# Attention on one core: the row reciprocals' path (transpose, copy, store, broadcast load) is reordered

## The chip, the cores and the metric

The kernel runs on 1 core of one Trainium2 chip. The metric is the device time of one execution in microseconds (us). The core has TensorE (PE; its weight loads are listed as PEld), VectorE (DVE), ScalarE (ACT), GpSimd (POOL) and SyncE (SP), which here only issues DMAs. PSUM is the memory that TensorE writes to, in banks of 512 fp32 columns; SBUF is the working memory. Engines run their own instruction lists in order and wait for each other by semaphores.

## What is computed

```python
def _attn_ref(q, k, v):                      # B, H, S, D = 4, 8, 576, 64
    scores = scale * q @ k^T
    mask = (pos[:, None] // 64) >= (pos[None, :] // 64)     # causal in blocks of 64
    scores = where(mask, scores, -1e9); scores -= max(scores, -1)
    attn = exp(scores)
    attn = attn / (sum(attn, -1) + 1e-9)
    return attn @ v
...
x = attn_out.transpose(0, 2, 1, 3).reshape(2304, 512)
x = elu(x @ w_in) @ w_out                    # d_ff = 2048
x = x + top-1 mixture of 8 experts (d_ff = 1024), for the tokens whose skip score is positive
```

The change lies in attention alone. The two feed-forward stages follow after it and aren't touched.

## The kernel before, in words

Attention handles the 32 heads as 16 pairs; the two heads of a pair lie one above the other in the 128 partitions. The 576 rows of a head are four row tiles of 128 (u = 0 to 3) and a tail of 64; the two tails of a pair together are the fifth tile (u = 4, `LAST`). The scores of tile u go to PSUM (`s_ps`), VectorE takes their negated maxima (`row_max`, L332, L335), ScalarE writes the exponentials to `prob` with their row sums in `rowsum` (`exp`, L456), TensorE transposes `prob` into `t_ps` (`turn_pair`, `turn_head`, `turn_last`, `turn_corner`, all recorded at L533), VectorE copies the result to `pt` (L342, L350, L356, L363), and TensorE multiplies `pt` with v into `o_ps` (`values`, L584). `o_ps` has the head's columns in its partitions and the 576 rows in its columns, not yet divided by the row sums.

The division needs each row's reciprocal along the columns, the same in 64 partitions. It is made so: ScalarE adds 1e-9 to the nine columns of sums (`guard`, L463), VectorE takes the reciprocals (`recips`, L373, tile `recip`, 128 x 9), TensorE transposes them together with the corner of the last tile into columns 384 to 511 of bank 0 of `t_ps` (`turn_pair` of the next pair, u = 0), VectorE copies them to `r_rows` (9 x 128, L368), SyncE stores these rows to `recip_rows` in device memory (`store_recips`, L218) and loads them back, broadcast over 64 partitions each, with four DMAs to `r_sb` (`load_recips`, L224, L227). VectorE then multiplies `o_ps` with `r_sb` into `attn_sb` (`final`, L379), and SyncE stores that (`store`, L211).

Work is software-pipelined over pairs. All engines have a `step(kk, i)` for pair `now` = n, in which they also do late parts of `past` = n-1 and `older` = n-2 and the preparation of `after` = n+1. Steps for pairs 0, 1, 14 and 15 and two closing steps are unrolled, the others are in a loop with two steps per turn. Each engine's list in a step is fixed by hand:

- TensorE: scores 0 and 1 of now; head tiles u = 3 of past; second half of values of older; the transposes of q's, of the tails', and (after the scores of u = 2) of k's tiles of after (`prep`, L492, groups 0, 1, 2, into banks 0, 1, 0 of `t_ps`); `turn_last` of past (bank 1); scores 3; `turn_pair` u = 0 (bank 0, with past's corner and reciprocals) and u = 1 (bank 1); scores of the last tile; first half of values of past; head tiles u = 2.
- VectorE: maxima 0 and 1; copies of past's head tiles u = 3; `recips(past)`; `final(older)`; maxima 2; `turned_last`; maxima 3; `turned_corner` and the copy to `r_rows`; `turned_pair` 0 and 1; maxima of the last tile; copies of head tiles u = 2.
- ScalarE: exponentials 0 and 1; copies of q's, the tails' and k's transposes to `qk_f` (`prep_copy`, L437, L442 and L444, L439); exponentials 2, 3 and last; `guard`.
- SyncE: load v (3 DMAs); store `attn_sb` of older; store the rows of past; load q and k of pair n+3 (6 DMAs); load `r_sb` of past (4 DMAs); load a piece of w_in.
- GpSimd splits q and k of after into high and low parts, then w_in's piece.

Where a text gives times inside a step, the reader can find each group by its line, operation and tile.

## Time and profile before

| | us |
|---|---|
| median of 3 runs | 856.7 (855.65 to 857.85) |
| the profiled execution | 859.39 |
| its span, first to last instruction | 857.7 |
| PE busy in the span | 804.7 (94%) |
| DVE busy | 531.8 (62%) |
| ACT busy | 340.1 (40%) |
| POOL busy | 241.4 (28%) |
| mean granted TensorE clock, share of full | 0.983 |

Attention takes the first 224 us of the span. The kernel behind it is on TensorE. Busy shares of the whole span are means over stages with different limits, so attention has to be read by itself, in its own windows: which engine waits there, for whom, and what stands behind the waiting instruction in its list. Idle time of an engine that isn't the bound costs nothing. Ends of matmuls are modelled, and their starts are the safer number. "Idle before <- releaser" is inferred from semaphore events.

### The profile page before, as it was taken

To read this page: it belongs to the slowest core of one execution; us is meant where nothing else is said; L and a number is where in the kernel's file an instruction comes from. 1 tells how busy PE (TensorE), PEld (TensorE's weight loads), DVE (VectorE), ACT (ScalarE), POOL (GpSimd) and SP (SyncE) were. 2 spreads that over 40 slices of the span, in tenths; PEclk is the share of its full clock that TensorE was granted. 3 is DMA by queue.
4 is the path that set the end of the run, shared out by engine and by line. 5 is a ranking of instruction groups with operands and counts; after the bars stand their busy time and mean duration, and the time that the engine had idled before them with its cause. 6 is when DMAs were issued, how large, how long until landed. Compare 5 with 4: busy or idle time off the path is not lost.

```text
span 857.7 us, 14746 instructions
## 1 busy us (share of the span) xinstructions
PE 804.7 (94%) x4618; PEld 665.6 (78%) x4619; DVE 531.8 (62%) x1318; ACT 340.1 (40%) x815; POOL 241.4 (28%) x232
## 2 busy tenths in 40 slices
PE   5998899999599999999999999999997999999995
PEld 4665666666598998898898888888985777887884
DVE  3766667677333358758848848843765799376342
ACT  3655546554133232232232222222443387255141
POOL 2756556554254202102102102100011233122121
PEclk9999999999699999999999999999999899999998
DMA  6344544553422421120021020050241599355100
GB/s 144 101 120 134 143 126 132 147 156 96 153 63 72 145 84 31 47 83 20 10 75 28 9 75 1 26 195 3 79 160 57 169 308 352 143 179 178 31 26 8
DMA packets 102913, 88.10 MB, mean 103 GB/s; under 512 B 66676, under 2 KB 78340, under 8 KB 102736
## 3 DMA queue, kind: packets, MB, share of 16 engines
q1 hardware_dynamic: 99808, 82.48, 31.1%
q0 software_dynamic: 3056, 5.00, 1.8%
q8 instruction: 26, 0.43, 0.2%
q14 instruction: 23, 0.19, 0.1%
HBM read 72.26 MB, written 18.34 MB: 106 GB/s over the span
## 4 chain that ended last, share of the span: by engine, by line
PE 69%; DVE 2%; issue 1%; DVEq 1%; ACT 0%; POOL 0%; POOLq 0%; ACTq 0%
PE h_ps L1563 11%; PE out_ps L1563 11%; PE h_ps L1564 11%; PE h_ps L1565 11%; PE out_ps L1565 11%; PE out_ps L1564 11%; PE out_ps L1698 1%; PE tr_ps L1663 1%; PE lg_ps L1614 1%; DVEq L864 0%; DVE xt_lo L1271 0%; PE tr_ps L1603 0%; DVE ht_lo L1310 0%; DVE x2t L1300 0%; DVE tile_ids L1280 0%
## 5 line engine op out<-in xcount | busy, mean ns | idle before, releaser
L1401 ACT ACTIVATE ex<-h_ps 128x384 f32<-128x384 f32 x96 | 47.2, 492 | 278.1 <-PE h_ps L1565 278.1
L1563 PE MATMUL h_ps<-xt_hi,wi_hi 128*128 128x384 f32 x384 | 133.4, 347 | 8.2 <-DVE xt_lo L1271 8.2
L1564 PE MATMUL h_ps<-xt_lo,wi_hi 128*128 128x384 f32 x384 | 131.4, 342 | 0.0
L1565 PE MATMUL h_ps<-xt_hi,wi_lo 128*128 128x384 f32 x384 | 131.2, 342 | 0.0
L1239 DVE TENSOR_SCALAR ex<-ex 128x384 f32<-128x384 f32 x96 | 34.8, 363 | 146.7 <-ACT ex L1401 145.6
L1563 PE MATMUL out_ps<-wo_hi,gt 128*128 128x512 f32 x288 | 114.6, 398 | 0.0
L1565 PE MATMUL out_ps<-wo_hi,gt 128*128 128x512 f32 x288 | 113.9, 395 | 0.0
L1564 PE MATMUL out_ps<-wo_lo,gt 128*128 128x512 f32 x288 | 113.3, 393 | 0.0
L456 ACT ACTIVATE prob<-s_ps,negmax 128x128 f32<-128x128 f32 (+2 forms) x144 | 77.9, 548 | 83.9 <-DVE negmax L332 74.3
L1121 DVE CUSTOM_DVE_ANT_0 x2t<-x,w_raw 128x512 bf16<-128x512 f32 x108 | 82.8, 807 | 0.4
L1563 PEld LDWEIGHTS h_ps<-xt_hi,wi_hi 128*128 128x128 f32 x384 | 73.3, 191 | 12.2 <-DVE xt_lo L1271 8.8
L1564 PEld LDWEIGHTS h_ps<-xt_lo,wi_hi 128*128 128x128 f32 x384 | 73.5, 191 | 3.1
L533 PE MATMUL t_ps<-ident,prob 128*128 128x128 f32 (+1 forms) x400 | 61.0, 284 | 15.1 <-DVE pt L356 14.4
L1565 PEld LDWEIGHTS h_ps<-xt_hi,wi_lo 128*128 128x128 f32 x384 | 73.4, 191 | 0.0
L1027 POOL DMA_INDIRECT route_table<-entry,slot x18 | 20.9, 1164 | 177.2 <-DVE slot L1200 161.0
L1019 POOL TENSOR_TENSOR xt_lo<-x_raw,xt_hi 128x384 fp32r<-128x384 f32 x20 | 28.4, 1419 | 142.7 <-ACT xt_hi L1415 142.6
L533 PEld LDWEIGHTS t_ps<-ident,prob 128*128 128x128 f32 (+1 forms) x400 | 42.2, 140 | 29.7 <-DVE pt L356 17.6
L1565 PEld LDWEIGHTS out_ps<-wo_hi,gt 128*128 128x128 f32 x288 | 54.1, 188 | 13.4
L1563 PEld LDWEIGHTS out_ps<-wo_hi,gt 128*128 128x128 f32 x288 | 54.1, 188 | 9.2 <-DVE gt L1232 0.8
L1564 PEld LDWEIGHTS out_ps<-wo_lo,gt 128*128 128x128 f32 x288 | 54.1, 188 | 8.9
L332 DVE TENSOR_REDUCE negmax<-s_ps 128x2 f32<-128x256 f32 (+1 forms) x64 | 51.1, 819 | 11.7 <-PE s_ps L528 11.5
L293 POOL TENSOR_TENSOR qk_hi<-qk_f,one 128x512 fp32r<-128x512 f32 (+1 forms) x30 | 36.0, 1199 | 79.1 <-PE s_ps L528 58.7
(174 smaller groups left out, 1647.1 us busy)
## 6 DMA issues: line engine op xcount, KB each, us to landing
w_raw<-in_moe_w_dram SPq DMA_DIRECT2D x56, 512.0 KB, 5.6
attn_t<-attn_sb SPq DMA_DIRECT2D x16, 288.0 KB, 2.1
x_raw<-attn_t SPq DMA_DIRECT2D x24, 192.0 KB, 2.7
out_dram<-x SPq DMA_DIRECT2D x18, 256.0 KB, 2.2
x_rows<-x SPq DMA_DIRECT2D x18, 256.0 KB, 2.5
raw_qk<-in_q_dram SPq DMA_DIRECT2D x32, 128.0 KB, 2.4
raw_qk<-in_k_dram SPq DMA_DIRECT2D x32, 128.0 KB, 2.4
v<-in_v_dram SPq DMA_DIRECT2D x32, 128.0 KB, 2.7
```

The lines of the kernel that those rows point to most:

```text
L293: pool.tensor_tensor(qk_hi[i][:, a:b], qk_f[i][:, a:b], one[:, :].to_broadcast([P, b - a]), ALU.mult).then_inc(split_hi, 1)
L332: dve.tensor_reduce(heads_cols(negmax, u), s_pair(u), AX_X, ALU.max, negate=True).then_inc(max_done, 1)
L456: act.activation(dst, src, ACT.Exp, bias=negmax[:, c:c + 1], accum_out=rowsum[i][:, c:c + 1]).then_inc(exp_done, 1)
L533: return pe.transpose(t_ps[0:src.shape[1], bank, at:at + P], src, ident[:, :])
L1019: pool.tensor_tensor(xtk(b % 2, 1, k), x_raw[k][:, :], xtk(b % 2, 0, k).bitcast(F32), ALU.subtract).then_inc(x_lo_done, 1)
L1027: pool.indirect_dma_start(table, bass.IndirectOffsetOnAxis(ap=slot[j][:, 0:1], axis=0), entry[j][:, :], None, bounds_check=E * N - 1, oob_ ...
L1121: ins = dve.tensor_tensor_reduce(dot_rows[:, ((E + 1) * t + e) % 2], x2[s][:, :], all_skip if e == E else all_gates[:, e, :], 1.0, 0.0, AL ...
L1239: dve.tensor_scalar(e, e, 1.0, -1.0, ALU.min, ALU.add).then_inc(em_done, 1)
L1401: act.activation(ex[:, f % 2], h_ps[:, f % 2, 0:NB], ACT.Exp).then_inc(ex_done, 1)
L1563: pe.matmul(dst, stat[0], mov[0], start=start, stop=False, skip_group_check=True)
L1564: pe.matmul(dst, stat[0], mov[1], start=False, stop=False, skip_group_check=True)
L1565: return pe.matmul(dst, stat[1], mov[0], start=False, stop=stop, skip_group_check=True)
```

## The change

The rows of reciprocals get a place of their own. TensorE transposes `recip` right behind the tails' transposes (`turn_recips`, into columns 128 to 255 of bank 1 of `t_ps`), for which it first waits for `rec_done`. ScalarE copies them to `r_rows` (`recip_rows`) between the copies of the tails' and of k's transposes; VectorE's copy is gone. The tails' `prep_copy` waits for the transposed reciprocals (`r_turned`) in place of the tails' own transposes, and `turn_last`, which overwrites bank 1, waits for ScalarE's copy (`r_row_done`). On SyncE the rows of past are stored ahead of `attn_sb` of older and loaded ahead of q and k. The rows in device memory are two buffers that alternate.

```diff
--- before.py
+++ after.py
@@ -75,9 +75,10 @@
     O0 = BANK - O_SPLIT
     COLS = 2 * FULL + 1
     TURNS = 7
+    R_LOADS = 64
     PIECES = [(j, max(j * P, a), b) for j in range(T) for a, b in ((0, O_SPLIT), (O_SPLIT, S)) if j * P < b]
     PARTS = [PIECES[0:4], PIECES[4:]]
-    R0 = BANK - P
+    R0 = P
 
     with ExitStack() as ctx:
         def sb(name, shape, dt):
@@ -108,7 +109,7 @@
         half_row = sb("half_row", [P, P], BF16)
         mask_row = sb("mask_row", [P, CAUSAL], BF16)
 
-        r_dram = nc.dram_tensor("recip_rows", (COLS, P), F32, kind="Internal").ap()
+        r_dram = [nc.dram_tensor(f"recip_rows{i}", (COLS, P), F32, kind="Internal").ap() for i in range(2)]
 
         s_ps = ctx.enter_context(nc.psum_tensor("s_ps", [P, 4 * BANK], F32))
         t_ps = ctx.enter_context(nc.psum_tensor("t_ps", [P, 2, BANK], F32))
@@ -128,6 +129,7 @@
         turned = sem("turned")
         guard_done = sem("guard_done")
         rec_done = sem("rec_done")
+        r_turned = sem("r_turned")
         r_row_done = sem("r_row_done")
         r_stored = sem("r_stored")
         r_in = sem("r_in")
@@ -211,20 +213,20 @@
                 sp.dma_start(attn_t[bass.ds((n % GROUP) * P, P), bass.ds((n // GROUP) * S, S)],
                              attn_sb[i][:, :]).then_inc(stored[i], 16)
 
-            def store_recips(n):
-
+            def store_recips(n, i):
 
                 wait(sp, r_row_done, n + 1)
-                sp.dma_start(r_dram, r_rows[:, :]).then_inc(r_stored, 16)
-
-            def load_recips(n):
+                sp.dma_start(r_dram[i], r_rows[:, :]).then_inc(r_stored, 16)
+
+            def load_recips(n, i):
+
                 wait(sp, r_stored, 16 * n + 16)
                 for h in range(2):
                     rows = slice(h * D, (h + 1) * D)
-                    sp.dma_start(r_sb[rows, 0:FULL * P], r_dram[h * FULL:(h + 1) * FULL, :]
+                    sp.dma_start(r_sb[rows, 0:FULL * P], r_dram[i][h * FULL:(h + 1) * FULL, :]
                                  .rearrange("(o u) q -> o (u q)", o=1).broadcast_to([D, FULL * P]))\
                       .then_inc(r_in, 16)
-                    sp.dma_start(r_sb[rows, FULL * P:S], r_dram[COLS - 1:COLS, rows]
+                    sp.dma_start(r_sb[rows, FULL * P:S], r_dram[i][COLS - 1:COLS, rows]
                                  .broadcast_to([D, TAIL])).then_inc(r_in, 16)
 
             def load_wi(n):
@@ -236,14 +238,14 @@
                 n, _ = pair(kk, i)
                 if not (isinstance(n, int) and n < 2):
                     load_v(n, i)
+                if (past := pair(kk, i, -1)):
+                    store_recips(*past)
                 if (older := pair(kk, i, -2)):
                     store(*older)
-                if (past := pair(kk, i, -1)):
-                    store_recips(past[0])
+                if past:
+                    load_recips(*past)
                 if (ahead := pair(kk, i, 3)):
                     load_qk(*ahead)
-                if past:
-                    load_recips(past[0])
                 if (after := pair(kk, i, 1)):
                     load_wi(after[0])
 
@@ -265,9 +267,9 @@
             for kk in (NK - 2, NK - 1):
                 for i in range(2):
                     step(kk, i)
+            store_recips(PAIRS - 1, 1)
             store(PAIRS - 2, 0)
-            store_recips(PAIRS - 1)
-            load_recips(PAIRS - 1)
+            load_recips(PAIRS - 1, 1)
             store(PAIRS - 1, 1)
             for i in range(2):
                 sp.wait_ge(stored[i], 16 * NK)
@@ -364,8 +366,6 @@
                                       t_ps[0:TAIL, 0, 2 * P:3 * P].rearrange("p (h w) -> p h w", h=2))
                 if last:
                     ins.then_inc(turned, 1)
-                wait(dve, r_stored, 16 * n)
-                dve.tensor_copy(r_rows[:, :], t_ps[0:COLS, 0, R0:R0 + P]).then_inc(r_row_done, 1)
 
             def recips(n):
 
@@ -374,7 +374,7 @@
 
             def final(n, i):
                 wait(dve, pv_done, n + 1)
-                wait(dve, r_in, 64 * n + 64)
+                wait(dve, r_in, R_LOADS * (n + 1))
                 wait(dve, stored[i], 16 * (n // 2))
                 dve.tensor_tensor(attn_sb[i][:, :], o_ps[:, O0:O0 + S], r_sb[:, :], ALU.mult)\
                    .then_inc(out_done, 1)
@@ -427,7 +427,11 @@
         def _(act):
             def prep_copy(n, i, g, bank):
 
-                wait(act, prep_t, 3 * n + g + 1)
+
+                if g == 1 and not (isinstance(n, int) and n < 2):
+                    wait(act, r_turned, n - 1)
+                else:
+                    wait(act, prep_t, 3 * n + g + 1)
                 if g == 0:
                     wait(act, split_lo, 2 * (n - 1))
                 if isinstance(n, int) and n == 0 and g == 0:
@@ -462,6 +466,12 @@
                 wait(act, rec_done, n)
                 act.activation(guarded[:, :], rowsum[i][:, :], ACT.Copy, bias=1e-9).then_inc(guard_done, 1)
 
+            def recip_rows(n):
+
+                wait(act, r_turned, n + 1)
+                wait(act, r_stored, 16 * n)
+                act.activation(r_rows[:, :], t_ps[0:COLS, 1, R0:R0 + P], ACT.Copy).then_inc(r_row_done, 1)
+
             for g in range(3):
                 prep_copy(0, 0, g, (0, 1, 0)[g])
 
@@ -473,6 +483,10 @@
                     if after:
                         prep_copy(*after, 0, 0)
                         prep_copy(*after, 1, 1)
+                if past:
+                    recip_rows(past[0])
+                if now:
+                    if after:
                         prep_copy(*after, 2, 0)
                     exp(*now, 2)
                     exp(*now, 3)
@@ -543,13 +557,11 @@
                         wait(pe, prep_out, 3 * ahead[0] + 3)
                     else:
                         wait(pe, turned, turns(n - 1, 3, 0))
-                    wait(pe, rec_done, n)
                 for h in range(2):
                     for j in range(c):
                         last = turn(u, (h * c + j) * P, prob[u][h][:, j * P:(j + 1) * P])
                 if u == 0 and past:
-                    turn(0, 2 * P, prob4[:, FULL * P:S])
-                    last = turn(0, R0, recip[:, :])
+                    last = turn(0, 2 * P, prob4[:, FULL * P:S])
                 last.then_inc(pt_done, 1)
 
             def turn_head(n, u, h):
@@ -560,9 +572,9 @@
                     last = turn(h, j * P, prob[u][h][:, j * P:(j + 1) * P])
                 last.then_inc(pt_done, 1)
 
-            def turn_last(n, ahead):
+            def turn_last(n):
                 wait(pe, exp_done, exps(n, LAST, 0))
-                wait(pe, *((prep_out, 3 * ahead[0] + 2) if ahead else (turned, turns(n, 3, 1))))
+                wait(pe, r_row_done, n + 1)
                 for j in range(FULL):
                     last = turn(1, j * P, prob4[:, j * P:(j + 1) * P])
                 last.then_inc(pt_done, 1)
@@ -570,9 +582,10 @@
             def turn_corner(n):
 
                 wait(pe, turned, turns(n, 3, 0))
-                wait(pe, rec_done, n + 1)
-                turn(0, 2 * P, prob4[:, FULL * P:S])
-                turn(0, R0, recip[:, :]).then_inc(pt_done, 1)
+                turn(0, 2 * P, prob4[:, FULL * P:S]).then_inc(pt_done, 1)
+
+            def turn_recips(n):
+                turn(1, R0, recip[:, :]).then_inc(r_turned, 1)
 
             def values(n, i, part):
                 wait(pe, turned, turns(n + 1, 0) if part else turns(n, LAST))
@@ -607,15 +620,20 @@
                 if after:
                     wait(pe, turned, turns(past[0], 3, 0)) if past else pe.wait_ge(prep_out, 3)
                     prep(*after, 0, 0)
-                    wait(pe, turned, turns(past[0], 3, 1)) if past else pe.wait_ge(prep_out, 3)
+                if past:
+                    wait(pe, turned, turns(past[0], 3, 1))
+                    wait(pe, rec_done, past[0] + 1)
+                if after:
                     prep(*after, 1, 1)
+                if past:
+                    turn_recips(past[0])
                 if now:
                     scores(*now, 2)
                 if after:
                     wait(pe, prep_out, 3 * after[0] + 1)
                     prep(*after, 2, 0)
                 if past:
-                    turn_last(past[0], after)
+                    turn_last(past[0])
                 if now:
                     scores(*now, 3)
                     turn_pair(now[0], 0, after, past)
```

## Rows read from the trace of the kernel before

**Rows 1.** Waits, 15:222 us: engine, tile, line <- releaser: us, times, longest

```profile
DVE attn_sb L379 <- DMA r_sb<-recip_rows: 33.4, 12, 3.5
...
PE t_ps L533 <- DVE pt L356: 14.4, 11, 1.9
```

**Rows 2.** VectorE's timeline: start, length, engine, line, tiles, [idle before <- releaser]

```profile
105.03 0.76 DVE L379 TENSOR_TENSOR attn_sb<-o_ps,r_sb 128x576 f32<-128x576 f32 x1 [2.81 <-DMA r_sb<-recip_rows]
...
108.50 0.27 DVE L368 COPY r_rows<-t_ps 9x128 f32<-9x128 f32 x1
...
114.90 0.20 DVE L373 RECIPROCAL recip<-guarded 128x9 f32<-128x9 f32 x1
118.22 0.76 DVE L379 TENSOR_TENSOR attn_sb<-o_ps,r_sb 128x576 f32<-128x576 f32 x1 [3.12 <-DMA r_sb<-recip_rows]
```

**Rows 3.** SyncE's DMA queue, timeline of the same step

```profile
108.79 0.31 SPq L218 DMA_DIRECT2D recip_rows<-r_rows  x1
109.42 0.97 SPq L195 DMA_DIRECT2D raw_qk<-in_q_dram  x2
...
113.31 0.51 SPq L224 DMA_DIRECT2D r_sb<-recip_rows  x1
...
115.14 0.60 SPq L227 DMA_DIRECT2D r_sb<-recip_rows  x1
...
117.02 0.93 SPq L195 DMA_DIRECT2D v<-in_v_dram  x2
118.13 0.69 SPq L197 DMA_DIRECT2D v<-in_v_dram  x1
```

**Rows 4.** Timeline of TensorE (matmuls), the stop in that step

```profile
120.50 0.66 PE L533 MATMUL t_ps<-ident,prob 128*128 128x128 f32 x4 [1.52 <-DVE pt L356]
121.25 0.40 PE L510 MATMUL s_ps<-qk_hi 128*128 128x288 f32 x1
```

**Rows 5.** VectorE's timeline, maxima opening three steps, and a final

```profile
34.13 1.02 DVE L332 TENSOR_REDUCE negmax<-s_ps 128x2 f32<-128x256 f32 x2 [0.23 <-PE s_ps L528]
...
190.02 1.02 DVE L332 TENSOR_REDUCE negmax<-s_ps 128x2 f32<-128x256 f32 x2 [0.24 <-PE s_ps L528]
...
192.28 0.70 DVE L379 TENSOR_TENSOR attn_sb<-o_ps,r_sb 128x576 f32<-128x576 f32 x1
...
201.09 1.02 DVE L332 TENSOR_REDUCE negmax<-s_ps 128x2 f32<-128x256 f32 x2 [0.23 <-PE s_ps L528]
```

**Rows 6.** Timeline of TensorE in the step from 188.98 us

```profile
194.06 0.63 PE L533 MATMUL t_ps<-ident,prob 128*128 128x128 f32 x4
194.62 0.50 PE L525 MATMUL s_ps<-qk_hi 64*128 64x512 f32 x2
...
196.05 0.60 PE L533 MATMUL t_ps<-ident,prob 128*128 128x128 f32 x4
196.41 0.38 PE L510 MATMUL s_ps<-qk_hi 128*128 128x288 f32 x1
```

**Rows 7.** SyncE's DMA queue, timeline after the last loads of q, k

```profile
197.31 0.30 SPq L218 DMA_DIRECT2D recip_rows<-r_rows  x1
199.57 0.45 SPq L224 DMA_DIRECT2D r_sb<-recip_rows  x1
...
215.17 0.29 SPq L218 DMA_DIRECT2D recip_rows<-r_rows  x1
216.40 0.45 SPq L224 DMA_DIRECT2D r_sb<-recip_rows  x1
```

**Rows 8.** Timeline of ScalarE in the step from 188.98 us

```profile
193.69 0.22 ACT L444 ACTIVATE qk_f<-t_ps 128x64 f32<-128x64 f32 x1
194.22 0.60 ACT L439 ACTIVATE qk_f<-t_ps 128x512 f32<-128x512 f32 x1 [0.30 <-PE t_ps L492]
```

**Rows 9.** The end of attention: timelines of TensorE and VectorE

```profile
214.81 2.92 PE L584 MATMUL o_ps<-pt,v 128*64 128x256 f32 x28 [0.78 <-DVE pt L356]
...
220.69 0.76 DVE L379 TENSOR_TENSOR attn_sb<-o_ps,r_sb 128x576 f32<-128x576 f32 x1 [5.55 <-issue]
```

## The prediction

> **What bounds the kernel now.** I read the list of waits over the attention stretch first. The DVE waits 33.4 us, in 12 of the 16 pairs, for the landing of `r_sb` before the multiply at L379 (`final`). TensorE waits 14.4 us, 11 times, for the copy at L356 (`turned_last`) [rows 1]. The second is the child of the first: in `step` of the DVE, `row_max(n, 2)` and `turned_last` stand behind `final`, and TensorE needs `turned_last` before it may reuse bank 1 of `t_ps` in `turn_pair(n, 1)`.
>
> Then I followed one pair in order of time. `final` starts at 105.03 and the next at 118.22, a step of 13.19 us [rows 2]. In between the chain closes on itself: `final` and the work queued behind it up to the copy of the reciprocals' rows (108.50, 0.27 long) [rows 2], SyncE's store of these rows at 108.79, the six loads of q and k from 109.42, the four broadcast loads of `r_sb` from 113.31 to 115.14 [rows 3], and the landing, 3.08 us after the last issue began. So the step is a latency loop through SyncE's queue, with 3.89 us of q's and k's issues (109.42 to 113.31) inside it. TensorE is not its bound: it stands 1.52 us before `turn_pair(n, 1)` and then needs 0.75 us to the next group (120.50 to 121.25) [rows 4].
>
> Where SyncE has no q and k left to load, the loop is gone, and the trace shows what the step is without it. The pair of maxima that opens a step stands at 34.13, 190.02 and 201.09 us [rows 5]. The 12 steps between the first two hold the 12 waits: 155.89 us, 12.99 each. The step from 190.02 to 201.09 has a `final` that doesn't wait and takes 11.07 us (its `final` starts at 192.28). There TensorE goes from one group to the next: `turn_pair(n, 1)` at 196.05 is followed by `scores(n, 4)` at 196.41, 0.36 later and not 0.75 [rows 6].
>
> **The change part by part.** All times t below are from the first score of that unstalled step (188.98, 1.04 us ahead of its maxima).
>
> 1. Order on SyncE. The rows' store and the four `r_sb` loads now go ahead of q's and k's. The rows are ready early in the step (below, t = 5.3). The store to its readers' issue takes 1.23 us (215.17 to 216.40) or 2.26 us (197.31 to 199.57), the only two kinds that the trace shows with nothing between [rows 7]. The last of the four issues starts 1.83 us after the first (113.31 to 115.14) [rows 3], and the landing ends 3.08 us after that (to 118.22 [rows 2]). So `r_sb` is in by t = 5.3 + 2.26 + 1.83 + 3.08 = 12.5 at the worse value. The `final` that wants it comes at t = 14.6 (in the unstalled step it starts 3.3 us after the first score [rows 5], and one step of 11.3 is added). The wait of 33.4 us goes, with 2.1 us to spare. `r_sb` is one buffer: its reload stands behind `store(older)`, which waits for `final(older)`; that one is done at t = 4.0, before the rows are even stored. Gain: 12 x (12.99 - 11.07) = 23.0 us.
>
> 2. TensorE. One transpose of `recip` (9 columns) leaves `turn_pair(n, 0)` and stands behind the tail of q and k: the same 0.12 us, earlier. Its new wait for `rec_done` comes before `prep(after, 1, 1)`. The reciprocal (0.20 long) follows the two copies of head 3 at once (114.90 to 115.10) [rows 2], the tail's transpose started 0.2 us after its end, so this wait costs 0.0 to 0.1 us. Behind it stand all later scores.
>
> 3. ScalarE. `recip_rows` is one more copy, 9 x 128 from PSUM, behind the tail copies, which end at t = 4.93 (193.69 + 0.22) [rows 8]. Its length lies between the 0.22 us of 64 columns and the 0.60 of 512 [rows 8]; by the slope between them 0.28. The bounds are 0.22 and 0.37 (an exponential of 128 columns). So the rows are in `r_rows` at t = 5.2, in the loop, where ScalarE runs 0.1 later, at 5.3. Behind it are queued `prep_copy(after, 2, 0)`, which could start at 5.24 before (194.22) [rows 8] because its transposes ended then, and now at about 5.35, and the exponentials of u = 2, which the `scores(n, 4)` wait for with 0.5 us to spare: covered.
>
> 4. `turn_last` now waits for `r_row_done`, not for the tail's copy. It stood at t = 5.08 (194.06) and was followed after 0.56 us [rows 6]. Now it is released at 5.2 to 5.3, and a group that TensorE had to stop for is followed by the next about 0.75 us after the release [rows 4]: the scores of u = 3 start at about 6.05 and not at 5.64, 0.4 late; one transpose less in `turn_pair(n, 0)` gives 0.12 back. The bounds are 0 (the release comes in time and nothing is refilled) and 0.45 (the longer copy and two waits). I take 0.25 us per step, nearer the stopped group, in the 12 steps and in three others that did not stall: 15 x 0.25 = 3.7 us lost.
>
> 5. VectorE loses the row copy, 0.27 us a step, behind which only its own copies stood. With no wait it has 2 us of room in a step of 11.3: nothing gained.
>
> 6. The end of attention. Pair 15's rows are now turned after its reciprocal (at 213.1) and not in the last corner. Before, their store went out at 215.17 [rows 7], and `final(15)` at 220.69 ended the stage [rows 9]. With ScalarE's copy done at 213.8 the store goes out at about 213.85, and all behind it moves with it: 1.3 us earlier, 219.4. TensorE's last multiplications (214.81, 2.92 us) [rows 9] come 0.5 later, as `turn_last` waits for the copy, and end at 218.3: covered. Gain 1.3 us.
>
> Sum: 23.0 - 3.7 + 1.3 = 20.6 us; I take 20.3, since the looped steps have 0.03 us more of loop edges than the unrolled one. The profiled execution took 859.4 (span 857.7); it would take 839.1. It lies 2.7 above the median of the runs, 856.7, and I carry the difference over: **836.4 us**. The rest of the kernel starts 20 us earlier and is otherwise the same.
>
> **The rivals.**
> SyncE becomes the bound. Its round in the loop: 7.60 us from the first load of q to the first of v (109.42 to 117.02), 1.80 for v (to 118.13 + 0.69) [rows 3], and from the store of rows to the loads of `r_sb` 1.23 to 2.26 us [rows 7], in which `store(older)` hides. That is 10.6 to 11.7 us against TensorE's 11.3: a near tie. At 11.7 it falls back 0.34 us a step, 4.1 in twelve, of which the 2.1 to spare absorb half: 838.4, still in the forecast. The new order stores the rows behind three loads of v, and none of the rows shows the store's latency there; at 3.0 us the round is 12.4 and the loss 12 x 1.1 - 2.1 = 11.1: 847.5. The Trainium skill (DMA: Bandwidth & Descriptors, Latency and other measured facts) says that HBM access takes 0.2 us on average but 2 us at high load and is the main part of a DMA's fixed cost; by it the store would take up to 1.23 + 1.8 = 3.0 us (an estimate), which would make this rival the forecast. The shown 1.23 and 2.26 us were in stretches with few loads, so no row here refutes it.
>
> **Slower**: the same place, but a store that takes 4.5 us. SyncE's round is then 13.9 us, 2.6 over TensorE's; 12 x 2.6 - 2.1 = 29.1 lost on the forecast: 865.5. It decides from about 4.0 us of store latency on (slower by over 0.3%). Against it: the longest seen is 2.26. For it: only this order makes the loads of q and k wait on that latency as well.
>
> The wait moves to TensorE. If the chain reciprocal, transpose, ScalarE's copy, `turn_last` runs 1 us later than I think (ScalarE held by late exponentials), each of 15 steps pays it: 851. Against it: the tail's copies end at t = 4.93 [rows 8] and the transpose of `recip` is done at about 4.0, so that the copy has both its inputs when its turn comes.
>
> The change does nothing: `final` still waits as long, because something other than q's and k's issues holds the loads. 857. Against it: [rows 2, 3] close the loop without a gap.
>
> **How the numbers follow.** Forecast 0.74; SyncE the bound (840 to 850) 0.12; TensorE's new wait (844 to 852) 0.06; nothing 0.03; slower 0.05. What a measurement of this kernel can tell from no change is about 0.3%, 2.6 us. Faster 0.74 + 0.12 + 0.06 = 0.92, same 0.03, slower 0.05. The forecast's own range: 0 and 0.45 us in point 4 give 832.6 and 839.4, the tail 1 us either way, the slower store 2.0: 831.5 to 842, which also holds the near part of the SyncE rival and leaves out less than 2 in 10.
>
> **What would show it.** Right: no `final` waits for a DMA; opening maxima 11.2 to 11.5 us apart; a short pause of TensorE before `turn_last` with ScalarE's row copy as its releaser; last `final` about 1.3 us sooner relative to the last step; SyncE waiting for `r_stored` 1 to 2 us a step. Wrong: `final` again idle for `r_sb` from some step on (SyncE), the wait before `turn_last` near 1 us (ScalarE), or a lower granted clock in the steps, which now run on TensorE's pace and would pay for it.

## The result, and the profile after

The changed kernel takes 835.85 us (median of 4 runs, 833.40 to 837.19) against 857.03 us before (4 runs): ratio 0.9751, 95% interval 0.9722 to 0.9781. The forecast was 836.4, range 831.5 to 842.0. Run again beside another kernel it took 838.85 us (5 runs, 836.47 to 840.13; before 857.15; ratio 0.978, 0.9756 to 0.9805). The two profiled executions of the changed kernel differ by 3.2 us in attention too (205.14 and 208.38 us to the first multiplication of the feed-forward), while the kernel before had nearly the same median both times; this is taken up below.

| one profiled execution each, us | before | after |
|---|---|---|
| its time | 859.39 | 834.67 |
| span | 857.7 | 833.0 |
| start of the span to the first multiplication of the feed-forward | 225.43 | 205.14 |
| from there to the end of the span | 632.3 | 627.9 |
| 12 steps from the opening maxima of pair 2 | 155.89 | 135.44 |

VectorE's timeline of two looped steps after (start, length, engine, line, operation, tiles, [idle before, releaser]; lines of the changed kernel differ by a few from before), which answers [rows 2, 5]:

```profile
101.41 1.02 DVE L334 TENSOR_REDUCE negmax<-s_ps 128x2 f32<-128x256 f32 x2 [0.23 <-PE s_ps L542]
...
103.80 0.76 DVE L379 TENSOR_TENSOR attn_sb<-o_ps,r_sb 128x576 f32<-128x576 f32 x1
...
112.60 1.02 DVE L334 TENSOR_REDUCE negmax<-s_ps 128x2 f32<-128x256 f32 x2 [0.24 <-PE s_ps L542]
...
114.99 0.76 DVE L379 TENSOR_TENSOR attn_sb<-o_ps,r_sb 128x576 f32<-128x576 f32 x1
```

The maxima that open a step are 11.19 us apart, and `final` has no idle time ahead of it. TensorE in the same step, around `turn_last` (105.68) and `turn_pair` with u = 0 and 1 (107.18, now seven transposes in a row), which answers [rows 4, 6]:

```profile
105.68 0.63 PE L547 MATMUL t_ps<-ident,prob 128*128 128x128 f32 x4
106.24 0.50 PE L539 MATMUL s_ps<-qk_hi 64*128 64x512 f32 x2
...
107.18 0.98 PE L547 MATMUL t_ps<-ident,prob 128*128 128x128 f32 x7
107.92 0.38 PE L524 MATMUL s_ps<-qk_hi 128*128 128x288 f32 x1
```

No line has an idle mark. ScalarE's last small copy of the tail and the new copy of the rows:

```profile
105.17 0.23 ACT L448 ACTIVATE qk_f<-t_ps 128x64 f32<-128x64 f32 x1
105.29 0.25 ACT L473 ACTIVATE r_rows<-t_ps 9x128 f32<-9x128 f32 x1
```

One step of the twelve is different. VectorE's timeline there:

```profile
161.94 0.76 DVE L379 TENSOR_TENSOR attn_sb<-o_ps,r_sb 128x576 f32<-128x576 f32 x1 [2.23 <-DMA r_sb<-recip_rows]
...
169.68 1.02 DVE L334 TENSOR_REDUCE negmax<-s_ps 128x2 f32<-128x256 f32 x2 [0.24 <-PE s_ps L542]
```

`final` again waits 2.23 us for `r_sb`, and the step that begins at 157.37 lasts 12.31 us.

### The profile page after: what moved, and what is told of

It reads as the page before. It is cut to its first block, busy times and chain, and to the rows that moved or that the text cites. A ratio compares the mean times of both kernels' runs of the same rounds, so it can differ in the third digit from the quotient of the medians.

```text
span 833.0 us, 14746 instructions
## 1 busy us (share of the span) xinstructions
PE 796.2 (96%) x4618; PEld 661.5 (79%) x4619; DVE 533.0 (64%) x1302; ACT 341.8 (41%) x831; POOL 241.5 (29%) x232
## 4 chain that ended last, share of the span: by engine, by line
PE 71%; DVE 2%; issue 1%; ACT 0%; DVEq 0%; POOL 0%; POOLq 0%; ACTq 0%
PE out_ps L1581 12%; PE h_ps L1581 11%; PE out_ps L1583 11%; PE out_ps L1582 11%; PE h_ps L1582 11%; PE h_ps L1583 11%; PE out_ps L1716 1%; PE tr_ps L1681 1%; PE lg_ps L1632 1%; DVE xt_lo L1289 0%; DVE ht_lo L1328 0%; PE tr_ps L1621 0%; DVE x2t L1318 0%; DVE xt_hi L1287 0%; ACT wi_hi L1471 0%
## 5 line engine op out<-in xcount | busy, mean ns | idle before, releaser
L547 PE MATMUL t_ps<-ident,prob 128*128 128x128 f32 (+1 forms) x400 | 57.7, 281 | 1.5 <-DVE pt L358 0.5
L1260 DVE TENSOR_TENSOR ex<-h_ps,ex 128x384 f32<-128x384 f32 x96 | 53.5, 558 | 3.3
L1581 PE MATMUL out_ps<-wo_hi,ht_hi 128*128 128x512 f32 x120 | 51.5, 429 | 4.0 <-DVE ht_lo L1328 3.8
```

What stands on the lines that cost most here:

```text
L547: return pe.transpose(t_ps[0:src.shape[1], bank, at:at + P], src, ident[:, :])
L1260: dve.tensor_tensor(e, h_ps[:, f % 2, 0:NB], e, ALU.max).then_inc(g_done, 1)
L1581: pe.matmul(dst, stat[0], mov[0], start=start, stop=False, skip_group_check=True)
```

## The experiments

**Which part carries the gain.** First the old order on SyncE with all the rest of the change (run `e1_old_queue`):

```diff
-                if (past := pair(kk, i, -1)):
-                    store_recips(*past)
                 if (older := pair(kk, i, -2)):
                     store(*older)
-                if past:
-                    load_recips(*past)
+                if (past := pair(kk, i, -1)):
+                    store_recips(*past)
                 if (ahead := pair(kk, i, 3)):
                     load_qk(*ahead)
+                if past:
+                    load_recips(*past)
```

> The changed kernel with SyncE's old order: attn_sb's store, the rows' store, q and k, and then the four r_sb loads. TensorE, ScalarE and VectorE as changed, so the rows are ready 5.2 us into the step instead of 8.3. Either-half theory (mine): the old loop was only 2 us longer than TensorE's list, so taking 3 us of waiting for rows out of it is enough by itself. From final to final the loop is then 0.76 + store 0.6 + rows' store 0.6 + q and k 3.9 + r_sb issues 1.8 + landing 3.1 = 10.8 us, under the 11.19 us step of the changed kernel: step about 11.2, time 835 to 839. Queue theory: q's and k's issues must leave the loop, or final waits on: step 12.5 or more, time 850 or more.

Measured: 836.21 us, ratio 0.9754 (0.9728 to 0.9781); the first multiplication of the feed-forward at 206.0. Its list of waits, and VectorE's timeline of one step:

```profile
DVE attn_sb L379 <- DMA r_sb<-recip_rows: 11.4, 12, 2.1
```

```profile
92.03 1.02 DVE L334 TENSOR_REDUCE negmax<-s_ps 128x2 f32<-128x256 f32 x2 [0.24 <-PE s_ps L542]
...
95.07 0.76 DVE L379 TENSOR_TENSOR attn_sb<-o_ps,r_sb 128x576 f32<-128x576 f32 x1 [0.70 <-DMA r_sb<-recip_rows]
...
103.22 1.02 DVE L334 TENSOR_REDUCE negmax<-s_ps 128x2 f32<-128x256 f32 x2 [0.23 <-PE s_ps L542]
```

`final` does wait in 12 steps, 11.4 us in all, and yet the step is 11.19 us (two are longer, 12.15 and 11.79, where the waits are 2.08 and 1.72). The others, of 0.4 to 1.1 us, lie in VectorE's spare time. The queue theory is wrong: q's and k's issues need not leave the loop.

Then the opposite, the kernel before with only SyncE's new order and the two buffers in memory (run `e2_queue_only`):

```diff
-                if (older := pair(kk, i, -2)):
-                    store(*older)
                 if (past := pair(kk, i, -1)):
-                    store_recips(past[0])
+                    store_recips(*past)
+                if (older := pair(kk, i, -2)):
+                    store(*older)
+                if past:
+                    load_recips(*past)
                 if (ahead := pair(kk, i, 3)):
                     load_qk(*ahead)
-                if past:
-                    load_recips(past[0])
```

> The kernel before with only SyncE's new order and the two row buffers in memory; reciprocals are transposed with the corner and copied by VectorE, as before. Either-half theory: rows ready at 8.3 us of the step, stored and loaded at once, r_sb in at 14.5 to 15.5, wanted at 14.4 with 0.66 us that VectorE idles anyway: step 11.1 to 11.5, time 833 to 840, perhaps under the changed kernel, since TensorE has no new wait. Early-rows theory: without the early rows the new order waits for the rows in front of everything, SyncE's round grows and the step stays at 12.5 or more, time 850 or more.

Measured: 841.82 us, ratio 0.983 (0.9795 to 0.9864); feed-forward from 210.9. Faster than before, so the early-rows theory is wrong as well, but 1.8 us over what I gave it. The list of waits:

```profile
DVE attn_sb L379 <- DMA r_sb<-recip_rows: 16.7, 12, 4.1
```

Its shortest steps take 11.10 us (there `final` waits 0.2 to 1.0 us, in VectorE's spare time), and the average from pair 4 to pair 13 is 11.41, which is SyncE's round here (the rows' stores from 53.68 to 145.10 us are 11.43 apart). The step with `x_raw`'s loads takes 15.79. Each half is enough to open the old loop, which was only 2 us longer than TensorE's list; the early rows alone bring all of it (836.21 us), the order alone about 15 of 21 us.

**Is SyncE at its limit?** In the changed kernel the rows are in `r_rows` at 105.54, and those of the next pair at 116.73, but SyncE's timeline shows that the store of the latter goes out 1.9 us late and that the queue hardly stands still:

```profile
116.87 0.93 SPq L197 DMA_DIRECT2D v<-in_v_dram  x2
...
118.64 0.50 SPq L219 DMA_DIRECT2D recip_rows<-r_rows  x1
119.61 0.39 SPq L213 DMA_DIRECT2D attn_t<-attn_sb  x1
120.83 0.49 SPq L226 DMA_DIRECT2D r_sb<-recip_rows  x1
```

Its stores of rows at 118.64 and, two pairs on, 141.43 are 11.40 us apart, in a stretch in which the step is 11.19. One more small issue a step (run `e5_one_more`):

```diff
                 if (ahead := pair(kk, i, 3)):
                     load_qk(*ahead)
+                if past:
+                    wait(sp, extra_in, 16 * past[0])
+                    sp.dma_start(extra[:, :], r_dram[past[1]][:, 0:D]).then_inc(extra_in, 16)
```

> The changed kernel with one more small DMA issue (9 rows of 256 bytes from the rows in memory to a scratch tile) on SyncE in every step, behind q's and k's loads. SyncE's round in the changed kernel is 11.4 us by its trace (rows' stores at 118.64 and 141.43), 0.2 over the step of 11.19. If SyncE is at its limit: round 12.0 to 12.1, the spare time of r_sb is used up after 2 to 3 steps, and from then on final waits and the step is the round: 12.0, time 7 to 9 us longer than the changed kernel, 842 to 845. If SyncE has room (it waits for r_stored in nearly every step, 9.9 us in all): the step stays 11.2 and the time within 1 us of the changed kernel.

Measured: 844.93 us, ratio 0.9861 (0.9835 to 0.9887). Steps of 11.2 to 11.3 for the first three, then 11.85 on average, and the rows' stores 11.84 apart; the step with `x_raw`'s loads takes 15.06. VectorE's and SyncE's waits:

```profile
DVE attn_sb L385 <- DMA r_sb<-recip_rows: 19.3, 10, 3.8
```

```profile
SPq L228 <- DMA recip_rows<-r_rows: 11.5, 15, 2.4
```

SyncE was at its limit: 9.1 us more than the 835.85 of the changed kernel, and 6.1 more than its 838.85, for a transfer of 2.25 KB that nobody needs. Waiting 11.5 us for the store of rows is no room, since that store is inside its round.

Fewer issues should then do the reverse. My first attempt loaded `r_sb` with two DMAs, each for both heads (run `e6_two_loads`):

```diff
-                for h in range(2):
-                    rows = slice(h * D, (h + 1) * D)
-                    ... (four loads of 64 partitions)
+                sp.dma_start(r_sb[:, 0:FULL * P], r_dram[i][0:2 * FULL, :]
+                             .rearrange("(h u) q -> h (u q)", h=2).unsqueeze(1)
+                             .broadcast_to([2, D, FULL * P])).then_inc(r_in, 16)
+                sp.dma_start(r_sb[:, FULL * P:S], r_dram[i][COLS - 1:COLS, :]
+                             .rearrange("o (h q) -> (o h) q", h=2).unsqueeze(1)
+                             .broadcast_to([2, D, TAIL])).then_inc(r_in, 16)
```

> The changed kernel with two loads of r_sb instead of four: each covers the 64 partitions of both heads. Same bytes. SyncE's round falls by 1.2 us to 10.2. If SyncE was at its limit (0.2 us a step behind, made up by the spare time until the loads of x_raw in the step at 157 us): the wait of 2.23 us for r_sb there goes, that step takes 11.1 instead of 12.3, and at the end of attention r_sb lands 1.2 to 2 us sooner; the other steps stay 11.19. Time 2 to 3 us under the changed kernel, 833 to 834. If SyncE had room: only the end of attention gains, 1.2 us.

Measured: 878.63 us, ratio 1.0264 (1.023 to 1.0298). Both theories missed. SyncE's timeline:

```profile
101.86 0.58 SPq L224 DMA_DIRECT2D r_sb<-recip_rows  x1
102.48 0.54 SPq L227 DMA_DIRECT2D r_sb<-recip_rows  x1
103.35 3.65 SPq L197 DMA_DIRECT2D raw_qk<-in_q_dram  x2
107.20 2.38 SPq L199 DMA_DIRECT2D raw_tail<-in_q_dram  x1
```

The two loads are issued in 0.6 us each, but q's that follow take 3.65 us for two and the tail's 2.38, against 0.98 and 0.69 in the changed kernel; VectorE waits 43.6 us for `r_sb` in 12 steps. The suspicion fell on the leading dimension of 2. The same four loads of 64 partitions as in the changed kernel, with the large ones described as 2 x 32 partitions (run `e10_split_64`):

```diff
-                                 .rearrange("(o u) q -> o (u q)", o=1).broadcast_to([D, FULL * P]))\
+                                 .rearrange("(o u) q -> o (u q)", o=1).unsqueeze(0)
+                                 .broadcast_to([2, D // 2, FULL * P]))\
```

> The changed kernel with its four loads of r_sb, same bytes, same 64 partitions each; only the two large loads are described with an outer dimension of 2 (2 x 32 partitions x 512) where the changed kernel has 64 (64 x 512). If the wide loads of the run with two loads were slow because their outermost count is 2, so that few of the 16 DMA engines carry them: the same here, q's loads stretched beyond 1.5 us for two, final waiting for r_sb by 1 us or more in most steps, 845 to 880 us. If they were slow because one DMA covered 128 partitions or 256 KB: nothing changes, 834 to 838.

Measured: 868.19 us, ratio 1.0141 (1.0115 to 1.0167). SyncE's timeline, and the `final` of that step:

```profile
112.35 0.48 SPq L230 DMA_DIRECT2D r_sb<-recip_rows  x1
...
114.32 1.38 SPq L199 DMA_DIRECT2D raw_tail<-in_q_dram  x1
115.80 1.64 SPq L197 DMA_DIRECT2D raw_qk<-in_k_dram  x2
```

```profile
119.37 0.76 DVE L380 TENSOR_TENSOR attn_sb<-o_ps,r_sb 128x576 f32<-128x576 f32 x1 [2.85 <-DMA r_sb<-recip_rows]
```

`final` waits 39.4 us for `r_sb` in 12 steps. The loads themselves land late: 7.0 us after the last of them begins to be issued (112.35 to 119.37), where the changed kernel's take 2.4 to 2.8 us. With 2.8 us this `final` would not have waited, since VectorE was free for it at 116.5. At the end of attention, where no load of q or k stands behind them, it is the same: 7.3 us from the last issue to `final`, against 2.68 in the changed kernel.

```profile
225.94 0.47 SPq L230 DMA_DIRECT2D r_sb<-recip_rows  x1
```

```profile
233.22 0.76 DVE L380 TENSOR_TENSOR attn_sb<-o_ps,r_sb 128x576 f32<-128x576 f32 x1 [8.59 <-issue]
```

The issues of q and k behind the loads stretch as well, to about 1.4 us for one and 1.6 for two. Same bytes, same partitions, same count: the shape of the description alone costs 29 to 32 us. The Trainium skill (DMA: Bandwidth & Descriptors, Why a DMA increments its semaphore by 16 and not by 1) has the rule: the largest number up to 16 that divides the slowest dimension of both sides is the number of DMA engines that carry the transfer, so 2 here and 16 with 64 outermost. The trace doesn't name the single engines, but it agrees in two ways. At that end of attention the 128 packets of 2048 bytes of the two large loads are under way from 225.6 to 232.4 us, never more than 4 at once; in the changed kernel from 196.1 to 199.5, up to 13 at once. And SyncE's queue has 448 packets less for the same bytes, 14 for each of the 32 large loads (16 less 2). The queue's line in the changed kernel's page and in this one's (packets, MB, share):

```profile
q1 hardware_dynamic: 99808, 82.48, 32.0%
```

```profile
q1 hardware_dynamic: 99360, 82.48, 30.7%
```

The run with two loads has 98848, 960 less: 64 loads at 16 against 32 loads at 2.

One issue less with 64 partitions outermost everywhere: the rows are kept as 2 x 576 in memory, stored with two DMAs and loaded with two (run `e7_one_less`):

```diff
-                sp.dma_start(r_dram[i], r_rows[:, :]).then_inc(r_stored, 16)
+                sp.dma_start(r_dram[i][:, 0:FULL * P].rearrange("h (u q) -> h u q", q=P),
+                             r_rows[0:2 * FULL, :]).then_inc(r_stored, 16)
+                sp.dma_start(r_dram[i][:, FULL * P:S], r_rows[COLS - 1:COLS, :]).then_inc(r_stored, 16)
...
+                for h in range(2):
+                    sp.dma_start(r_sb[h * D:(h + 1) * D, :], r_dram[i][h:h + 1, :].broadcast_to([D, S]))\
+                      .then_inc(r_in, 16)
```

> The counterpart of the run with one more issue: rows in memory are kept as 2 x 576, stored with two DMAs (eight rows, and the ninth) and loaded with two of 64 partitions x 576 each, so four issues a step and not five. Every load still spreads over 64 partitions of one head. If SyncE is at its limit with a round of 11.4: round 10.8 when it isn't held, it now waits for its inputs, the spare time of r_sb stays, the wait of 2.23 us near 160 us falls under 0.5, that step takes 11.1 to 11.5; the end of attention gains 0.6 to 1.2 us; time 1 to 2 us under the changed kernel, about 834. If loads to 64 partitions with 2304 bytes each stretch later issues as the two wide loads did (3.65 us for two of q's): 850 or more.

Measured: 833.73 us, ratio 0.9723 (0.9703 to 0.9744). No `final` waits for `r_sb`, the step with `x_raw`'s loads takes 11.19 like the others, and the feed-forward starts at 203.8. SyncE's waits (releaser: us, times, longest):

```profile
SPq L197 <- PE o_ps L595: 7.7, 10, 1.5
SPq L227 <- DMA recip_rows<-r_rows: 4.3, 6, 1.0
```

It now waits for TensorE's `values` in 10 steps before it may load v: it is held by the step and no longer behind it. Its last `final` starts 18.87 us after the last maxima, 0.55 sooner than in the changed kernel (0.6 to 1.2 were expected). Again, beside the changed kernel itself on the same chip (runs `e7_again` and `after_again`):

> The kernel with four issues for the rows instead of five, once more. With SyncE's round 0.6 us shorter it waits for TensorE and not TensorE for it: attention 203.6 to 203.9 us as before, no wait for r_sb before the last pair; median 1.5 to 3 us under the changed kernel of the same call, 833 to 835. If the gain of the first run was chance: same medians within 0.5 us.

> The changed kernel itself once more, beside the next one on the same chip. Its attention, from the span's start to the first multiplication of the feed-forward, took 205.1 us in the first profile. The run with pair 14's store moved has the same loop and yet took 208.5, after one store of rows that needed 4.0 us to its readers. If SyncE's round stands at the edge of the step, the changed kernel itself varies so: 204 to 209, medians 835 to 838. If that came from the moved store: 205.0 to 205.3.

Measured: 834.07 us, ratio 0.9739 (0.972 to 0.9758), against 838.85, ratio 0.978 (0.9756 to 0.9805), for the changed kernel. In this execution the changed kernel's attention took 208.4 us and not 205.1:

```profile
DVE attn_sb L379 <- DMA r_sb<-recip_rows: 5.5, 5, 3.7
```

Five waits for `r_sb` and not one, with 3.65 us in the step with `x_raw`'s loads, which takes 15.33 us. Not all of that is waiting: TensorE stops for 1.95 us, and then its granted clock falls to half (1.2 GHz) for 3.4 us. TensorE's timeline, and the stretch behind the stop (columns: window, length, busy time and instructions of PE, PEld, DVE, ACT and POOL, granted clock, DMA share, GB/s):

```profile
166.10 0.66 PE L547 MATMUL t_ps<-ident,prob 128*128 128x128 f32 x4 [1.95 <-DVE pt L358]
```

```profile
166.10:171.10 5.00, 4.91 (x26) 3.04 (x26) 2.85 (x5) 3.19 (x11) 2.94 (x3) 0.66 0.63 177
```

In the first profile the stop in this step was 0.52 us and the clock stayed full. At half speed 3.4 us of time are 1.7 us of work lost (an estimate), so that the stop and the clock together are most of the 4.1 us over a step of 11.19. The same step shows the same fall in `e2_queue_only`, `e4_tail_store` and `e5_one_more`, behind stops of 2.1 to 2.5 us.

The kernel with one issue less started its feed-forward at 203.1 and 203.8 in its two profiles. It is the fastest version tried, by 4.8 us side by side with the changed kernel and by 2.1 over the first sets of runs.

**Two smaller things.** `x_raw`'s loads later (run `e3_x_later`):

```diff
+            for kk in (NK - 2, NK - 1):
+                if kk == NK - 1:
+                    for i in range(2):
+                        sp.wait_ge(stored[i], 16 * (GROUP // 2))
+                    for c in range(len(x_raw)):
+                        load_x_rows(sp, attn_t, c, 0, x_raw, x_in)
-            for kk in (NK - 2, NK - 1):
                 for i in range(2):
```

> The changed kernel with the four loads of x_raw on SyncE moved from ahead of the step of pair 12 to ahead of that of pair 14, where there are no more loads of q and k. In the changed kernel one step of fourteen takes 12.31 us and not 11.19, with a wait of 2.23 us for r_sb. If these four issues (1.83 us of queue) are its cause: that step takes 11.1 to 11.4, its final waits 0 to 0.4 us for r_sb, attention is 0.8 to 1.2 us shorter by the trace, and the steps before are the same. If it is the last straw of a queue that had been falling behind anyway: the wait comes in the same step, of 1.5 us or more. The time moves by 1 us at most, which the runs can't tell apart: the trace decides.

Measured: 834.9 us, ratio 0.9737 (0.9716 to 0.9758). The step takes 11.20 and its `final` waits 0.76; the feed-forward starts at 203.9 and not 205.1. The five finals before it wait 0.20 to 0.55, so SyncE is as far behind as in the second profile of the changed kernel, but those waits cost nothing. The four loads are what made a wait that costs. They do it twice: by 1.8 us of issues, and by the store of rows behind them, whose loads go out 2.80 us after it (154.46 to 157.26) where one step earlier it was 2.08. With the loads moved it is 2.04 there. SyncE's timeline in the changed kernel around them:

```profile
141.43 0.50 SPq L219 DMA_DIRECT2D recip_rows<-r_rows  x1
...
150.94 1.79 SPq L31 DMA_DIRECT2D x_raw<-attn_t  x4
...
154.46 0.51 SPq L219 DMA_DIRECT2D recip_rows<-r_rows  x1
...
157.26 0.50 SPq L226 DMA_DIRECT2D r_sb<-recip_rows  x1
...
159.09 0.60 SPq L229 DMA_DIRECT2D r_sb<-recip_rows  x1
```

The last store of `attn_sb` behind the last `r_sb` loads (run `e4_tail_store`):

```diff
-            store(PAIRS - 2, 0)
+            wait(sp, out_done, PAIRS - 1)
             load_recips(PAIRS - 1, 1)
+            store(PAIRS - 2, 0)
```

> The changed kernel with pair 14's attn_sb store on SyncE behind the last four r_sb loads and no longer ahead of them. In the changed kernel one of these issues takes 1.53 us and not 0.60, which eats 0.93 of the 1.27 us by which the rows' store came earlier. If the 288 KB store that is in flight stretches it: issues of 0.6 us each, the last final about 0.9 us sooner after the last maxima (18.5 us and not 19.42). If the stretching comes from something else: it stays at 19.3 to 19.5. The time moves by 1 us at most.

Measured: 836.52 us, ratio 0.9752 (0.9729 to 0.9775). The last `final` starts 19.13 us after the last maxima, 0.29 sooner than in the changed kernel and not the 0.9 that the store in flight would have given; the stretched issue is shorter but still there:

```profile
197.47 0.29 SPq L219 DMA_DIRECT2D recip_rows<-r_rows  x1
198.74 0.44 SPq L226 DMA_DIRECT2D r_sb<-recip_rows  x1
199.22 1.29 SPq L229 DMA_DIRECT2D r_sb<-recip_rows  x1
```

So the store in flight isn't its main cause, and what is stays open. The loop of this kernel is word for word that of the changed one, and still it ran differently: ten `final`s waited 0.8 to 3.8 us, from pair 2 on. The first trouble is one store of rows:

```profile
51.70 0.50 SPq L219 DMA_DIRECT2D recip_rows<-r_rows  x1
52.68 0.39 SPq L213 DMA_DIRECT2D attn_t<-attn_sb  x1
55.68 0.49 SPq L226 DMA_DIRECT2D r_sb<-recip_rows  x1
```

From 51.70 to the loads that wait for it at 55.68 are 4.0 us, where 1.2 to 2.4 is usual. The store of the same pair took long in two other runs as well: 3.8 us in `e5_one_more` and 3.6 in `e6_two_loads`, but 2.1 in the changed kernel.

All three changes together (run `e9_combined`):

> All three: one issue less, x_raw's loads later, the last attn_sb store behind the last r_sb loads. If each cause is as stated, steps of 11.1 to 11.2 throughout, no wait for r_sb before the last pair, the last final 1 to 1.5 us sooner after the last maxima; together 2 to 3 us under the changed kernel: 833 to 834, ratio to the kernel before 0.972 to 0.973.

Measured: 836.03 us, ratio 0.9748 (0.9729 to 0.9767); attention 203.65 us, the last `final` 19.15 us after the last maxima. The forecast of 833 to 834 missed: the last `final` came 0.27 us sooner than in the changed kernel, and not 1 to 1.5. The three changes give attention no more than one issue less alone, and the median is 2.3 us above that of `e7_one_less`; I would keep the simpler kernel.

## Why the prediction was right, point by point

**The bound** was read rightly. With the loop opened, the step fell from 12.99 to 11.19 us, and 11.07 to 11.11 us is what it takes in unrolled steps before and after. No other engine took over at once.

**Point 1** (the wait goes, "with 2.1 us to spare"): the gain was right, the spare time wasn't. I let SyncE store the rows the moment that they are ready, t = 5.3. They were ready at t = 5.2 (105.54 less the step's first score at 100.37). But the store for the next pair went out at 118.64 although its rows were ready at 116.73, since SyncE was still at v. Its round is 11.40 us, within the 10.6 to 11.7 that the rival had given it, and 0.2 over the step; that is why each pair used up a little of the spare time. The rival "SyncE becomes the bound" was therefore the right mechanism, present and nearly harmless in 12 steps, at one step's cost. Of that one step I had no term at all: the loads of `x_raw`, 1.8 us of issues (150.94), pushed the rows' store from its turn to 154.46, and the step cost 1.12 us in the first profile and 4.1 in the second, there with the fall of the clock. A lower granted clock was among my signs of being wrong; in the looped steps it didn't come, in this one it did. I had read SyncE's queue in the looped step and left out what the unrolled part adds to it. I had also put the whole 23.0 us down to the order on SyncE. `e1_old_queue` shows that this isn't so: with q's and k's issues still ahead of the `r_sb` loads, the rows that are ready early (my points 2 and 3) bring the same time, and the order alone brings 15 us.

**Point 4** (0.25 us a step for `turn_last`): 0.12 was measured, 11.19 against 11.07, and 0.09 against the 11.10 of looped steps without the new wait (`e2_queue_only`). The release came where I had it: ScalarE's copy took 0.25 us (0.28 expected, bounds 0.22 to 0.37) and ended at 105.54, t = 5.17. TensorE started `turn_last` at 105.68, and the next group came 0.56 us later and not 0.75. The step that failed is "a group that TensorE had to stop for is followed by the next about 0.75 us after the release" [rows 4]: that row is of a stop of 1.5 us, this one was 0.1 after TensorE's own pace. Of the three other steps that I had also charged with 0.25, the two that can be compared paid 0.04 (11.03 and 11.11 us).

**Point 2 and 3**: right. The tail's transpose is 3.57 us after the first score in both kernels, so `rec_done` costs nothing.

**Point 6** (1.3 us at the end of attention): nothing came of it. SyncE's timeline, which answers [rows 7]:

```profile
193.60 0.29 SPq L219 DMA_DIRECT2D recip_rows<-r_rows  x1
...
194.82 0.46 SPq L226 DMA_DIRECT2D r_sb<-recip_rows  x1
195.32 1.53 SPq L229 DMA_DIRECT2D r_sb<-recip_rows  x1
...
197.53 0.60 SPq L229 DMA_DIRECT2D r_sb<-recip_rows  x1
```

and VectorE's, which answers [rows 9]:

```profile
200.21 0.76 DVE L379 TENSOR_TENSOR attn_sb<-o_ps,r_sb 128x576 f32<-128x576 f32 x1 [4.95 <-issue]
```

The rows' store is 1.27 us earlier, 12.81 after the last maxima (180.79) and not 14.08. Then one issue takes 1.53 us and not 0.60, and the landing 2.68 and not 2.52: the `final` is 0.18 earlier, and the first multiplication of the feed-forward, 24.35 us after the last maxima, is where it was (24.34).

**The sum.** Expected for attention 20.3 us, measured in the first profile 20.29. The exact match is luck: 1.6 us too much taken off in point 4 (12 x 0.13) and about 0.6 in the three steps beside them stand against 1.3 that didn't come at the end and 1.1 for `x_raw`. The second profile gives 17.1 us. The two medians of the changed kernel, 835.85 and 838.85, lie on both sides of the 836.4. Of the signs that I had named for being right, SyncE's wait for `r_stored` was shorter than said: 9.9 us in 13 steps, 0.8 a step and not 1 to 2.

**The rest of the kernel**, "otherwise the same", was 4.4 us shorter in the profile. Nothing ties this to the change. Both kernels start the feed-forward at a granted clock of half, after 7 us without TensorE:

```profile
225.43:300.00 74.57, 74.07 (x356) 67.10 (x357) 26.75 (x56) 25.63 (x54) 30.02 (x22) 0.94 0.36 112
```

```profile
205.14:280.00 74.86, 74.42 (x366) 66.77 (x367) 29.17 (x59) 26.58 (x57) 29.22 (x22) 0.97 0.35 111
```

(columns: window, length, busy time and instructions of each engine, granted clock, DMA share, GB/s.) The kernel before ran 9.3 us of it at that level (1.2 GHz), the changed one 4.5. The 4.8 us between them are worth about 2.4 (an estimate: half of it); the other 2 us are no more than the spread among the kernels with the same feed-forward. In those the time at half was 3.0 to 6.1 us and the stretch from the first multiplication to the end 627.2 to 630.6, and in `e3_x_later` 9.2 and 631.9. That my carrying over the difference of profile and median comes out by the medians is luck as well: it rested on the new profiled execution lying 2.7 us above its median like the old one, and it (834.67) lay 1.2 below, 4.4 under the 839.1 that I gave it.

**The slower rival**: a store latency of over 4.0 us in every step. Once 4.0 was seen, in one step of `e4_tail_store`. The Trainium skill's figure for a loaded memory (DMA: Bandwidth & Descriptors, Latency and other measured facts), from which 3.0 us would have come, isn't what the usual steps show: 1.2 to 2.4 us in the new place too. About that much, 2.8 to 3.2 us, stood only behind `x_raw`'s four loads, in both profiles of the changed kernel. `final` was never held by it for good. "TensorE's new wait" and "the change does nothing" did not happen.

## What to carry to other kernels

Where an engine waits once in a loop, write out the loop's length through every queue and compare it with the list of the engine that will be next: here they were 13.0 and 11.1, so one edit that takes the loop below the list brings the whole gain (the early rows), another most of it (the order, 15 of 21 us), and both together bring spare time and not more speed. Then count the issuing queue's own round the same way, with what is issued outside of the loop's body: a round 0.2 us over the step hardly shows in twelve steps and leaves the kernel sensitive to a single late store and to four more loads. In such a queue the number of issues counts and not the bytes: one of 2.25 KB more cost 6 to 9 us, one less gained 2 to 5.

## What was not expected of the hardware

The outermost dimension in these loads' description decided their speed: 64 x 512 against 2 x 32 x 512 elements, same destination and bytes, is 836 to 839 against 868 us. The loads land 7 us after the last issue and not 2.7, and the issues of other loads behind them stretch as well (0.69 to 1.4 us for one; with 2 x 64 x 512, 0.98 to 3.65 us for two).

Single issues of 0.6 us take 1.0 to 1.9 us now and then, mostly the second or third load of `r_sb`; the kernels with two loads of 64 x 576 (`e7_one_less`, `e7_again`, `e9_combined`) show none of these. What stretches them is open.

How long the granted clock stayed at half once TensorE worked again after a pause of 6.3 to 7.7 us varied from 3.0 to 9.3 us between executions, about 3 us of this kernel's time (an estimate: half of the difference).

A stop of TensorE of 2.0 to 2.5 us in the step with `x_raw`'s loads was followed by 3.4 us at half clock in four profiles out of four. The length of the stop alone doesn't decide it: behind stops of 2.1 and 2.4 us in two early steps of `e10_split_64` the clock stayed full.
